# A channel product by seven products of half blocks for eight, in one fused kernel

## Time and profile before

| | us |
|---|---|
| median of 3 runs | 524.54 |
| lowest, highest | 522.26, 524.54 |
| the profiled execution | 522.32 |
| its span, first to last instruction | 520.5 |

### The profile page before, as it was taken

How to read it: one execution, slowest core, us unless ns; L and a number is a source line. 1 busy time by engine, 2 the same in 40 slices (tenths; PEclk the granted TensorE clock), 3 DMA queues, 4 the chain that set the end, 5 groups by cost and what they waited for, 6 DMA issues and landing times.

```text
span 520.5 us, 7462 instructions
## 1 busy us (share of the span) xinstructions
PE 512.7 (99%) x2822; PEld 438.8 (84%) x2822; DVE 187.5 (36%) x530; ACT 182.9 (35%) x454; POOL 125.2 (24%) x120
## 2 busy tenths in 40 slices
PE   8999999999999999999999999999999999999997
PEld 7899789887888888888888888888888998889995
DVE  5666667411222513121112221111565246440440
ACT  7877787532223311121010242322443212331121
POOL 6885776244333300000000144342000000000000
PEclk9999999999999999999999999999999999999999
DMA  8812630022223200000000032230000000110002
GB/s 236 288 42 62 210 137 1 3 82 81 82 87 110 87 1 0 2 0 0 1 0 1 12 100 74 78 111 1 0 1 2 0 1 12 51 42 20 1 20 101
DMA packets 12244, 27.85 MB, mean 54 GB/s; under 512 B 2224, under 2 KB 2224, under 8 KB 12208
## 3 DMA queue, kind: packets, MB, share of 16 engines
q1 hardware_dynamic: 10336, 23.96, 14.2%
q10 hardware_dynamic: 1872, 3.41, 1.7%
HBM read 24.22 MB, written 3.15 MB: 53 GB/s over the span
## 4 chain that ended last, share of the span: by engine, by line
PE 94%; ACT 2%; POOL 2%; DMA 1%; issue 1%; DVE 0%; SPq 0%; ACTq 0%; POOLq 0%
PE bank L1002 28%; PE bank L1193 25%; PE bank L1181 25%; PE bank L1054 7%; PE bank L1022 3%; PE bank L1037 3%; PE bank L1061 1%; ACT prob L793 1%; POOL w_slot L423 1%; DMA qk_raw<-in_qk 1%; PE bank L1086 1%; PE bank L1075 1%; POOL qk_split L384 0%; ACT bias L781 0%; ACT bias L776 0%
## 5 line engine op out<-in xcount | busy, mean ns | idle before, releaser
L1193 PE MATMUL bank<-hid,w_slot 128*128 128x512 f32 x576 | 139.3, 391 | 0.0
L1181 PE MATMUL bank<-u_split,w_slot 128*128 128x512 f32 x576 | 138.5, 390 | 0.0
L1193 PEld LDWEIGHTS bank<-hid,w_slot 128*128 128x128 f32 x576 | 107.8, 188 | 23.1 <-issue 0.9
L1181 PEld LDWEIGHTS bank<-u_split,w_slot 128*128 128x128 f32 x576 | 107.9, 188 | 22.3
L659 DVE SCALAR_TENSOR_TENSOR hid<-bank,hid 128x512 fp32r<-128x512 f32 x48 | 33.2, 692 | 192.2 <-ACT hid L895 192.2
L895 ACT ACTIVATE hid<-bank 128x512 fp32r<-128x512 f32 x48 | 28.7, 599 | 203.4 <-PE bank L1181 203.4
L423 POOL TENSOR_TENSOR w_slot<-stage,w_slot 128x1024 fp32r<-128x1024 f32 x16 | 38.2, 2387 | 52.4 <-ACT w_slot L847 52.4
L1002 PE MATMUL bank<-sp_slot,vn 128*128 128x384 f32 x288 | 50.3, 335 | 0.0
L1002 PEld LDWEIGHTS bank<-sp_slot,vn 128*128 128x128 f32 x288 | 50.0, 188 | 0.2
L793 ACT ACTIVATE prob<-prob,row_min 128x256 f32<-128x256 f32 (+1 forms) x96 | 45.8, 479 | 10.9 <-DVE row_min L510 10.9
L1054 PEld LDWEIGHTS bank<-v_all,probT 128*128 128x128 f32 x352 | 41.8, 192 | 3.8 <-issue 1.4
(11 more groups left out here) (89 smaller groups left out, 467.0 us busy)
## 6 DMA issues: line engine op xcount, KB each, us to landing
stage<-in_w_ch SPq DMA_DIRECT2D x16, 512.0 KB, 3.3
qk_raw<-in_qk SPq DMA_DIRECT2D x23, 256.0 KB, 4.9
v_all<-in_v SPq DMA_DIRECT2D x12, 256.0 KB, 5.1
out_dram<-o_stage ACTq DMA_DIRECT2D x12, 256.0 KB, 2.0
stage<-in_w_spT SPq DMA_DIRECT2D x6, 384.0 KB, 3.0
stage<-in_w_in SPq DMA_DIRECT2D x4, 512.0 KB, 3.2
stage<-in_w_out SPq DMA_DIRECT2D x2, 512.0 KB, 3.5
V_raw<-in_V SPq DMA_DIRECT2D x4, 96.0 KB, 4.7
```

The costliest lines, as they stand in the source:

```text
L1181: last = mm(h_bank[g % 2][:], w_slot[f][:, a, k * P:(k + 1) * P], u_split[c][:, m, k, :], start=(k == 0 and p == 0), stop=(k == KD - 1 and ...
L1193: last = mm(c_ring[(KD * c + k) % 6][:], w_slot[f][:, a, 512 + k * P:512 + (k + 1) * P], hid[g % 2][:, m, :], start=(f == 0 and a == HI an ...
```

## The change

The first product is done for pairs of blocks (`PAIRS` = 8, so `G` = 24 periods). The weight matrix of a pair is cut in 2 x 2 blocks (two halves of the 512 input channels, two blocks of hidden channels), and u of a chunk in 2 x 2 blocks (the same halves, and two halves of 256 tokens). Seven products of such blocks or of sums of them give the four results (Strassen's scheme in Winograd's form). Each product is 2 slices x 3 passes = 6 matmuls of 256 columns.

The sums of weights and their split parts live in `comb`, two buffers that are remade for every pair in every chunk; w_ch1 is therefore loaded anew for each chunk. w_ch2 stays in slots of its own. The seven blocks of u per chunk are in `u_first` and `u_last`. Three banks hold the first products: `h_run` gathers P1, P6, P7, P4 in turn, with a copy taken by ScalarE (`keep`) between them; `h_two` holds P2, `h_three` P5 and then P3. VectorE adds kept parts to get three of the four results (`sum_h`). The contraction of the pair before is cut in four parts that stand between the later products. `c_ring` has 5 banks. Items and products of stage 3 stay; their tiles get other addresses.

The core of the diff (declarations, addresses and the branch for wide windows are left out; `...` marks cuts):

```diff
 SyncE
+            def load_w1(g):
+                if g >= 2:
+                    sp.wait_ge(comb_lo, 4 * (g - 1))
+                f = 2 * (g % PAIRS)
+                sp.dma_start(w1_raw[g % 2][:], w_ch[f:f + 2, :, 0:512].rearrange("f p w -> p f w")
+                             ).then_inc(w1_in[g % 2], 16)
...
 GpSimd, in its attention loop
-                    if g in (11, 13, 15):
-                        split_stage((g - 11) // 2)
-                    if g >= 17 and g % 2:
-                        split_u((g - 17) // 2)
+                    if g == 7:
+                        add_w(0, (0, 1))
+                    if g == 8:
+                        add_w(0, (2, 3))
+                    if 9 <= g < 13:
+                        split_w1(0, g - 9)
+                    if g in (13, 14):
+                        split_w2(g - 13)
+                    if g == 18:
+                        split_u(0)
+                        add_u(0)
+                    if g == 19:
+                        split_u(1)
+                        add_u(1)
...
+                    if g == 22:
+                        split_u(4)
+                        split_u(5)
+                    if g == 23:
+                        split_u(6)
 GpSimd, after it
-            for n in range(EARLY, STAGES):
+            add_w(1, range(4))
+            for g in range(1, G):
+                for n in range(4):
+                    split_w1(g, n)
+                if g < PAIRS:
+                    split_w2(2 * g)
+                    split_w2(2 * g + 1)
+                if g >= 2 * PAIRS + 3:
+                    split_stage(g - 2 * PAIRS - 3)
+            for n in range(PAIRS - 3, LATE):
                 split_stage(n)
 VectorE
+            def add_w(g):
+                r, half = w1_raw[g % 2], slice(0, 256)
+                dve.wait_ge(w1_in[g % 2], 16 * (g // 2 + 1))
+                dve.wait_ge(comb_lo, 4 * g)
+                vec.tensor_tensor(w_sums[:, 0, :], r[:, 1, half], r[:, 1, 256:512], ALU.add).then_inc(w_added, 1)
+                vec.tensor_tensor(w_sums[:, 2, :], r[:, 0, half], r[:, 1, half], ALU.subtract).then_inc(w_added, 1)
+                dve.wait_ge(w_added, 4 * g + 1)
+                vec.tensor_tensor(w_sums[:, 1, :], w_sums[:, 0, :], r[:, 0, half], ALU.subtract).then_inc(w_added, 1)
+                dve.wait_ge(w_added, 4 * g + 3)
+                vec.tensor_tensor(w_sums[:, 3, :], r[:, 0, 256:512], w_sums[:, 1, :], ALU.subtract
+                                  ).then_inc(w_added, 1)
...
             for g in range(G):
+                c, p = divmod(g, PAIRS)
+                if c and p == 0:
+                    for n in range(4, 7):
+                        split_u(c, n)
+                if c and p == 1:
                     for k in range(KD):
                         sum_y(KD * (c - 1) + k)
+                if 2 <= g + 1 < G:
+                    add_w(g + 1)
+                dve.wait_ge(ps_p2, g + 1)
+                sum_h(0, h_two, 0, (kept_p1, g + 1), sum_11)
+                low_h(g, 0, whole[0][:], 0, 0)
+                if g == 3:
+                    split_z(1)
+                dve.wait_ge(ps_p5, g + 1)
+                sum_h(1, h_three, 2, (kept_u3, g + 1), sum_22)
+                low_h(g, 1, whole[1][:], 1, 1)
+                if (g, 1) in MIX_AT:
+                    sum_u(MIX_AT[g, 1])
+                low_h(g, 2, h_run[:, 0:HC], 1, 0)
+                dve.wait_ge(kept_u2, g + 1)
+                sum_h(2, h_three, 1, (ps_p3, g + 1), sum_12)
+                low_h(g, 3, whole[2][:], 0, 1)
+                if (g, 3) in MIX_AT:
+                    sum_u(MIX_AT[g, 3])
+                if c < CH - 1 and p == 6:
+                    for n in range(2):
+                        add_u(c + 1, n)
+                    for n in range(2):
+                        split_u(c + 1, n)
+                if c < CH - 1 and p == 7:
+                    for n in range(2, 4):
+                        split_u(c + 1, n)
+                    for n in range(2, 4):
+                        add_u(c + 1, n)
+                if c == 2 and 2 <= p < 6:
+                    split_y(p - 2)
 ScalarE, in its attention loop
-                    if s in (16, 18, 20, 22):
-                        round_u((s - 16) // 2)
+                    if 17 <= s < 22:
+                        round_u(0, s - 17)
+                    if s == 22:
+                        round_u(0, 5)
+                        round_u(0, 6)
 ScalarE, channel mixing
+            for g in range(G):
+                c, p = divmod(g, PAIRS)
+                if g == 3:
+                    round_z(1)
+                keep(g, 0, ps_p1, sum_11, kept_p1)
+                if c and p == 0:
+                    for n in range(4, 7):
+                        round_u(c, n)
+                if g + 1 < G:
+                    round_blocks(g + 1)
+                high_h(g, whole[0][:], sum_11, 0, 0)
+                keep(g, 1, ps_p6, sum_12, kept_u2)
+                if g == 0:
+                    take_xT(TILES - 1)
+                if g + 1 < G:
+                    round_sums(g + 1)
+                keep(g, 2, ps_p7, sum_22, kept_u3)
+                high_h(g, whole[1][:], sum_22, 1, 1)
...
+                high_h(g, h_run[:, 0:HC], ps_p4, 1, 0)
+                high_h(g, whole[2][:], sum_12, 0, 1)
+                if g + 1 < PAIRS:
+                    round_w2(2 * g + 2)
+                    round_w2(2 * g + 3)
+                if c < CH - 1 and p == 6:
+                    for n in range(4):
+                        round_u(c + 1, n)
                 if c == 2:
+                    if 2 <= p < 6:
+                        round_y(p - 2)
+                    if 2 <= p:
+                        split_stage(p - 2)
 TensorE
+            def product_h(g, n, dst, start, stop, done):
...
+                for k in range(2):
+                    for q, (a, m) in enumerate(PASSES):
+                        last = mm(dst[:, 0:HC], comb[g % 2][:, a, w, k * P:(k + 1) * P], u[:, m, k, :],
+                                  start=(start and k == 0 and q == 0), stop=(stop and k == 1 and q == 2),
+                                  skip_group_check=True)
+                last.then_inc(done, 1)
...
+            def gap(g, i):
+                if g:
+                    contract(g - 1, i)
...
+            pe.wait_ge(x_half, QUADS)
+            for g in range(G):
+                pe.wait_ge(comb_lo, 4 * g + 4)
+                if g:
+                    pe.wait_ge(h_hi, 4 * g - 1)
+                    pe.wait_ge(h_lo, 4 * g - 1)
+                product_h(g, 0, h_run, True, True, ps_p1)
+                product_h(g, 1, h_two, True, True, ps_p2)
+                if g:
+                    pe.wait_ge(sum_12, g)
+                product_h(g, 2, h_three, True, True, ps_p5)
+                pe.wait_ge(kept_p1, g + 1)
+                product_h(g, 3, h_run, False, True, ps_p6)
+                gap(g, 0)
+                pe.wait_ge(kept_u2, g + 1)
+                product_h(g, 4, h_run, False, True, ps_p7)
+                gap(g, 1)
+                pe.wait_ge(kept_u3, g + 1)
+                product_h(g, 5, h_run, False, True, ps_p4)
+                gap(g, 2)
+                pe.wait_ge(sum_22, g + 1)
+                product_h(g, 6, h_three, False, True, ps_p3)
+                gap(g, 3)
```

## The result

The changed kernel takes 579.4 us (median of 4 runs, 574.6 to 580.1), the one before 523.4 in the same session: 1.105 times as long, 95% interval 1.099 to 1.111. The forecast was 566 with a range of 528 to 580. The profiled execution took 574.6 us, its span is 572.8 against 520.5 before, 52.3 more; it is the fastest one, with a mean granted clock of 0.975, and the others ran at 0.964 to 0.967.

What follows compares the result with a forecast made beforehand. TensorE's matmuls, busy 99% of a 520.5 us span, were taken as the bound. Terms: -9.6 + 3.4 + 2.4 + 15 + 23.3 + 9.1 = +43.6 on the profiled 522.3, so 565.9 us; range 528 to 580.

Steps and rivals of the forecast that it cites:

- Arithmetic: First product on TensorE: 1008 matmuls of 256 columns at 120 ns replace 576 of 512 columns, saving 9.6 us.
- Hand-over: From attention to the first product: late block scores, ScalarE rounding and last x_half cost 3.4 us (0 to 5).
- Pair 0: Pair 1's weights are summed late on GpSimd, so pair 1 starts 8.1 us after pair 0 against 5.7: 2.4 us.
- (a): Pairs 1 to 6: VectorE's sums of weights and GpSimd block each other, P7 2.5 us late each, 15 us.
- (b): Pairs 7 to 9 and 15 to 17: extra VectorE work ahead of the first sum makes P7 late, 23.3 us together.
- (c): Pairs 19 to 22: GpSimd's splits for later stages delay P7 by 3.05 us, three of four counted, 9.1 us.
- Clock in the pairs: Granted clock falling after long holes: only a condition that would put the time above the range, given no size.
- rival of 140 ns: TensorE's 256-column matmuls cost 140 ns and more, 20 us on top, 586 us; chance 0.07.
- 0.55 for ScalarE: Before the first product: one more rounding ahead of ScalarE's half of probT costs 0.55 us.
- upper bound of 3.1: Pairs 1 to 6: P7 is 3.1 us late in each if VectorE and GpSimd strictly alternate.
- main theory: The forecast itself, TensorE waiting at P7 in pairs 1 to 6, at chunk boundaries and in chunk 2: 565.9 us; chance 0.60.
- second rival: P7 is reached in time at all boundaries, only the hand-over cost stays, 516 us; chance 0.07.

Runs made afterwards that it cites:

- e4: Changed kernel with matmuls whose results nobody reads placed in TensorE's holes, every wait kept: 566.6 us, 1.085 of before.
- e1: Changed kernel with VectorE's sums of weights moved behind the first product's sum, and their ScalarE copy behind the third copy: 533.2 us, 1.022 of before.
- e2: Changed kernel with GpSimd's low parts of the second weights cut from 512 to 16 columns from block 2 on: 557.5 us, one run.
- e9: e7 with the sums of weights made once in chunk 0, stored to device memory and loaded back in chunks 1 and 2: 519.6 us, 0.9948 of before.
- e7: Changed kernel with its queue orders rewritten and repaired over several versions, sums of weights still made for every pair: 527.7 us, 1.012 of before.
- e6: Changed kernel reordered: chunk 0's u on GpSimd, other chunks' u over three pairs, stage split between GpSimd's weight splits: 530.8 us, 1.017 of before.
- e3: Changed kernel with GpSimd's first splits and sums of u one attention step later, behind the copies of the global keys: 574.9 us.

## Why the prediction was right, step by step

The wait was forecast in its place and nearly in its size; one term was missing, and that the time fell inside the range is luck. The profiled span grew by 52.3 us, the forecast for it was 43.6. In both, the lateness of P7 is its start after the pair's first product less 4.26, its start in a plain pair.

| Step | Forecast | Measured |
|---|---|---|
| Arithmetic | -9.6 | -7.7 (24 pairs at 10.56 for 10.88) |
| Hand-over | +3.4 | +3.3 (106.07 for 102.74), 0.9 of it the early half clock |
| Pair 0 | +2.4 | +2.4 (8.06 for 5.7 of work) |
| (a) pairs 1 to 6 | +15 | +13.8 (3.0, 2.4, 1.25, 2.4, 2.4, 2.3) |
| (b) chunk boundaries | +23.3 | +20.5 (4.7, 4.65, 2.0, 2.55, 4.65, 2.0) |
| (c) pairs 19 to 22 | +9.1 | +9.9 (four times 2.5) |
| Clock in the pairs | not in the sum | +10.1 (what is left; 9.3 of it found against e4) |

**The arithmetic.** 24 matmuls of 256 columns in 2.87 us, 120 ns each, as read off the line through the earlier trace rows. The rival of 140 ns is out. The Trainium skill's figure ("TensorE: Matmul & The Clock Gate", Back-to-back issue gap), 109 ns, was not reached here, where every matmul has its own weights; the page itself calls it the gap of an isolated matmul, without a budget for the weight load. The missing 1.9 us, 0.08 in each pair, don't lie in the short matmuls but in the second products, which the forecast left alone: cut in groups of six, these take 1.39 us a group (246.72 to 248.11 above), where six times 226.7 ns make 1.36. Why a group costs 0.03 us more is not shown.

**The hand-over** came out at 3.3 for 3.4 by luck. The scores were 0.8 and then 1.0 us late (0.8 and 1.25 forecast), the last x_half held P1 for 0.6 (0.8), and the 0.55 for ScalarE didn't show; that makes 2.4, as in e1, e2 and e4 (2.3 to 2.5). The rest is the half clock at 8.76 us.

**The mechanism.** The wait was named in the right place (ScalarE's second copy, behind VectorE's first sum, behind the sums of weights). For VectorE's trade with GpSimd I had two rows and took 2.5 us for each pair; four of six came to 2.3 to 2.4, and e2 shows the cause. That turns change strictly, even between VectorE's first two sums, which don't wait for each other, I had put at the upper bound of 3.1; in pair 4 above it is what happens, and the lateness is 2.4 all the same. The middle of my chain was thus wrong: the first two sums end 3.3 us after the first product, not at 2.2. The end of it was right, since the four GpSimd instructions in between take about the time that I had given them: the fourth sum ends at 5.6 for 5.4, and P7 starts at 6.67 for 6.75. The Trainium skill ("SBUF — State Buffer", SBUF: two separate sides) tells of the shared port; this trace agrees and adds the order of the turns. In (c) I had counted three of four pairs at 3.05 us; all four were late, by 2.5 each, and the two errors nearly cancel.

**The boundaries** all came out late in the right order, each 0.35 to 0.7 us less than forecast; which turn of GpSimd I had counted too many in each I did not trace.

**What was missing** is the clock. The prediction ends with "If the granted clock falls after the long holes, the time is above my range": I had it as a condition and gave it no term. It fell, six times in the pairs, and costs 10.1 us by the table and 9.3 pair by pair against e4. The waits were forecast at 53.2 us together and measured 49.9, the arithmetic gained 1.9 less than forecast, and the clock added 10.1: the profiled execution came out 8.7 us above the forecast's 565.9. The median lies 4.8 us higher still; by the mean clocks (0.967 for 0.975) the other executions spend some 9 us more at half clock, and I estimate half of that, 4.8, as the price. So the number came out 13 us low. The time is above the bracket that the prediction gives its main theory (550 to 578; the bounds named beside it, 0 to 3.1 a pair and 0 to 12.2, make it 542 to 573), and it stayed inside the wide range by 0.6 us only. The trace of before shows no hole in the steady stretch, so the size could only have been bounded: a matmul of 512 columns at half clock takes 427 ns for 227 (six from 224.29 to 226.85 in pair 8), for as long as the clock stays down.

The second rival (the cover holds, 516) named the right condition: sum_11 has to come early. e1 makes it hold in most pairs by order alone and lands at 533, not at 516, since the sums then press on what comes behind them; e9 lands at 520 when they are gone from two of three chunks.

## What to carry to other kernels

Where a change moves load from the engine that is the bound to its helpers, look at the first instruction there that the bound engine will wait for, and put the new work behind it: here the same instructions cost 56 us in front and 11 behind. A product taken off TensorE is worth only what the helpers can hide, so read their busy share by stage (VectorE and GpSimd had 59.8 and 52.0 us of 91 in pairs 0 to 6, as shown under e2, and 20.7 and 18.9 of 42.2 in four plain pairs, row below). Busy time holds the time lost to turns as well: of VectorE's 59.8 us, 20 went when GpSimd's long instructions did (e2). What is the same for each chunk was better kept in memory than made again (e9, 8.1 us under e7). And a hole on TensorE can be dearer than its length, as in six of the 16 pairs with a hole here: give the half clock behind it a term of its own.

```profile
244.00:286.20 42.20, 42.20 (x266) 38.10 (x265) 20.65 (x45) 18.13 (x40) 18.88 (x16) 1.00 0.16 51
```

## What the runs showed of the hardware

A GpSimd instruction gets in between two VectorE sums in SBUF that are queued back to back and don't depend on each other: in pair 4 L774 took 1.28 and L775 1.51 us in place of 0.42 each. The price of a turn is the length of GpSimd's instruction: 2.62 us for one sum beside a 128x1024 split (e6 at 329.80), 0.41 to 0.44 beside splits of 16 columns (e2 at 159.26).

The granted clock fell to 0.5 behind a hole of 2.73 us (pair 1) and of 4.49 (pair 8), and not behind that of 2.24 in pair 4. Behind the four holes of 2.3 us in pairs 19 to 22, which look alike, it fell twice (19 and 21) and stayed up twice. In e3 it fell behind the hole of 1.83 us in pair 17, which it passed in the changed kernel, and stayed up in pair 19. What decides stays open. With the holes filled by unread matmuls (e4) it stayed at 1.0 in all pairs of the profiled execution, also behind the one hole left open, of 2.33 us ahead of P6 in pair 7.
